# Sums of x for the last three tiles on VectorE in steps 54 to 61, and seven more high halves of weight products on ScalarE

## The reference

```python
# chunked local attention: q, k, v are (4, 8, 768, 64); chunks of 32 queries see 16 keys to the left, 8 to the right, and 8 memory keys
a = softmax(scale * q_c @ k_full.T); out[:, :, c] = a @ v_full
x = out.transpose(0, 2, 1, 3).reshape(3072, 512)
h = x @ w_in0; g = where(h > 0, h, exp(min(h, 0)) - 1); x = g @ w_out0      # layer 1: 512 -> 2048 -> 512
h = x @ w_in1; r = maximum(h, 0); g = s * r * r + b;    x = g @ w_out1      # layer 2, same sizes
```

## Time and profile before

| | us |
|---|---|
| median of three runs | 1180.54 |
| the profiled execution's own time | 1176.55 |
| its span, first to last instruction | 1174.8 |
| attention ahead of step 0 | 97 |
| tile 0 and tile 1 (attention woven in) | 97 to about 526 |
| tile 2, tile 3 | 526 to 688, 688 to 849 |
| tile 4, tile 5 | 849 to 1007, 1007 to 1163 |
| PE, DVE, ACT, POOL busy | 1107.5, 846.0, 769.7, 424.8 |

### The profile page before, as it was taken

How to read it: one execution, slowest core, us unless ns; L and a number is a source line. 1 busy time by engine, 2 the same in 40 slices (tenths; PEclk the granted TensorE clock), 3 DMA queues, 4 the chain that set the end, 5 groups by cost and what they waited for, 6 DMA issues and landing times.

```text
span 1174.8 us, 18155 instructions
## 1 busy us (share of the span) xinstructions
PE 1107.5 (94%) x5787; PEld 881.7 (75%) x5787; DVE 846.0 (72%) x1234; ACT 769.7 (66%) x1799; POOL 424.8 (36%) x458
## 2 busy tenths in 40 slices
PE   8999888988899999999999899998999999999998
PEld 4667566766687777778788687886887887878876
DVE  5786686369957956996948978839948459667385
ACT  4896676577667657757758567666666366675464
POOL 5788778651232332235265233655201001000000
PEclk9999989999999999999999899998999999999999
DMA  9998999999698789869899579996687666776664
GB/s 211 275 267 256 357 290 327 347 297 326 184 286 240 227 242 271 266 191 348 297 356 353 173 255 375 299 349 226 197 249 241 193 194 186 212 222 187 197 183 158
DMA packets 204055, 302.81 MB, mean 258 GB/s; under 512 B 112824, under 2 KB 121016, under 8 KB 203960
## 3 DMA queue, kind: packets, MB, share of 16 engines
q1 hardware_dynamic: 203960, 301.65, 83.8%
HBM read 226.10 MB, written 75.50 MB: 257 GB/s over the span
## 4 chain that ended last, share of the span: by engine, by line
PE 66%; DVE 6%; issue 4%; ACT 3%; DMA 3%; SPq 0%; POOL 0%; ACTq 0%; DVEq 0%; POOLq 0%
PE ps L1010 31%; PE ps L995 31%; DMA w_ring<-w_scratch 2%; ACT ps L1090 1%; DVE g_lo L1450 1%; PE ps L959 1%; DVE X L1367 1%; PE ps L907 1%; PE ps L932 1%; DVE att L1336 1%; DVE xc_lo L1360 1%; DMA elu<-x_scratch 1%; DMA w_raw<-in_moe_w_out 1%; DVE y L1367 1%; PE ps L901 0%
## 5 line engine op out<-in xcount | busy, mean ns | idle before, releaser
L1010 PE MATMUL ps<-g_hi,w_ring 128*128 128x512 f32 x1344 | 426.3, 399 | 22.3 <-issue 16.8
L995 PE MATMUL ps<-xc_hi,w_ring 128*128 128x512 f32 x1344 | 434.0, 396 | 8.4 <-ACT ps L1138 3.3
L1010 PEld LDWEIGHTS ps<-g_hi,w_ring 128*128 128x128 f32 x1344 | 253.5, 192 | 81.6 <-issue 22.4
L995 PEld LDWEIGHTS ps<-xc_hi,w_ring 128*128 128x128 f32 x1344 | 253.1, 188 | 65.4 <-DMA w_ring<-w_scratch 5.3
L1010 PE MATMUL ps<-g_lo,w_ring 128*128 128x512 f32 x672 | 265.1, 395 | 0.0
L995 PE MATMUL ps<-xc_lo,w_ring 128*128 128x512 f32 x672 | 262.4, 391 | 0.0
L782 POOL TENSOR_TENSOR w_new<-w_raw,w_new 128x256 fp32r<-128x256 f32 x182 | 162.4, 896 | 196.3 <-ACT w_new L1227 193.0
L1450 DVE TENSOR_TENSOR g_lo<-X,g_hi 128x512 fp32r<-128x512 f32 x240 | 186.4, 781 | 52.5 <-ACT g_hi L1213 52.0
L1213 ACT ACTIVATE g_hi<-X 128x512 fp32r<-128x512 f32 x240 | 148.8, 627 | 72.5 <-PE ps L1010 66.2
L1367 DVE TENSOR_TENSOR X<-s,ps 128x512 f32<-128x512 f32 x144 | 96.1, 681 | 93.1 <-ACT s L1150 68.5
L1010 PEld LDWEIGHTS ps<-g_lo,w_ring 128*128 128x128 f32 x672 | 128.4, 191 | 27.7
(11 more groups left out here) (116 smaller groups left out, 1388.4 us busy)
## 6 DMA issues: line engine op xcount, KB each, us to landing
w_ring<-w_scratch SPq DMA_DIRECT2D x336, 512.0 KB, 4.4
w_scratch<-w_new SPq DMA_DIRECT2D x182, 256.0 KB, 5.0
w_scratch<-att SPq DMA_DIRECT2D x42, 256.0 KB, 4.9
w_raw<-in_moe_w_in SPq DMA_DIRECT2D x16, 512.0 KB, 5.5
w_raw<-in_moe_w_out SPq DMA_DIRECT2D x16, 512.0 KB, 6.3
x_scratch<-y SPq DMA_DIRECT2D x12, 512.0 KB, 6.4
att<-x_scratch SPq DMA_DIRECT2D x12, 512.0 KB, 6.6
out<-elu SPq DMA_DIRECT2D x24, 256.0 KB, 4.4
```

What stands on the lines that cost most here:

```text
L995: last = nc.tensor.matmul(bank_of(st.pi, st.i), w[:, a, cols], x[:, st.pi, kk, :], start=(st.pi in (P1, P5, P4) and kk == 0 and n == 0), s ...
L1010: last = nc.tensor.matmul(bank_of(st.pi, d), w[:, a, cols], x[:, k % RING, :], start=(st.pi in (P1, P5) + (P4,) * (1 - st.gr) and st.i == ...
```

## The change

HEAD_PREP goes from 42 to 35, so ACT also makes the high halves of products 35 to 41, at steps 7, 7, 8, 9, 10, 11 and 12, and the seven rooms come into use seven products earlier. The slots of the later products are respaced: product 42 goes from step 12 to 13, 49 from 18 to 19, products 56 to 75 stay or move by one, 83 stays at 50, and from there they come up to two steps earlier, the last (111) at 78 instead of 80. The saves due before load d follow: for d = 4 to 9 they were 34, 36, 38, 40, 42, 42 and are 34, 35, 35, 37, 39, 41.

The 24 sums of x for tiles 3 to 5 go from POOL to DVE: in steps 54 to 61 of tiles 2, 3 and 4, one in a step, in the order P5, P7, P6, P4, kk = 0 and 1 in turn. P5 and P4 of kk = 1 get room of their own (`t_more`, 4 KB in each partition), so no sum overwrites a quarter that is still to be split. They stand on DVE behind what the step has otherwise, and in front of the woven attention. POOL then runs straight from set SETS + 4 to the last set.

```diff
-HEAD_PREP = 42
+HEAD_PREP = 35
...
-        return 12 + (pp - HEAD_PREP) * 19 // 20 + (3 if pp >= PREP_AT[PAIR + 1, P1] else 0)
+        return 7 + (pp - HEAD_PREP) * 9 // 10 + (3 if pp >= PREP_AT[PAIR + 1, P1] else 0)
...
+LATE_SUMS = 54
...
+        t_more = sb("t_more", [128, 2, HALF])
...
+        late_sums = sem("late_sums")
...
+        def late_sum(t, kk, pi):
+            return 8 * (t - TPL) + 2 * (SUM_T[pi] - 1) + kk + 1
...
-            if kk == 1 and pi == P6:
-                return t_late[:, 3, :]
+            if kk == 1 and pi in (P5, P6, P4):
+                return {P5: t_more[:, 0, :], P6: t_late[:, 3, :], P4: t_more[:, 1, :]}[pi]
...
-            for m in range(SETS + 4, SETS + 10):
+            for m in range(SETS + 4, 2 * SETS):
                 prepare((m,))
-            for kk in range(2):
-                sums_of_x(3, kk)
-            for m in range(SETS + 10, 2 * SETS):
-                prepare((m,))
-            for t in range(4, TILES):
-                for kk in range(2):
-                    sums_of_x(t, kk)
...
-                if pi not in (P1, P3, P2):
+                if t >= TPL and pi not in (P1, P3, P2):
+                    act.wait_ge(late_sums, late_sum(t, kk, pi))
+                elif pi not in (P1, P3, P2):
...
+            def late_x_sum(t, kk, pi):
+                x11, x12, x21, x22 = (x_from(t, kk, b) for b in (P1, P7, P2, P3))
+                t1, t2, t4 = (x_from(t, kk, b) for b in (P5, P6, P4))
+                if pi == P5:
+                    dve.wait_ge(x_in[kk], 32 * t)
+                    to, a, b = t1, x12, x11
+                elif pi == P7:
+                    dve.wait_ge(late_sums, late_sum(t, kk, P5))
+                    to, a, b = x12, x22, x12
+                elif pi == P6:
+                    dve.wait_ge(late_sums, late_sum(t, kk, P5))
+                    to, a, b = t2, x22, t1
+                else:
+                    dve.wait_ge(late_sums, late_sum(t, kk, P6))
+                    to, a, b = t4, x21, t2
+                nc.vector.tensor_tensor(to, a, b, ALU.subtract).then_inc(late_sums, 1)
...
+                t, s = divmod(g, PER_TILE)
+                if TPL <= t + 1 < TILES and 0 <= s - LATE_SUMS < 8:
+                    late_x_sum(t + 1, (s - LATE_SUMS) % 2, (P5, P7, P6, P4)[(s - LATE_SUMS) // 2])
```

More of the change, by code:

```diff
@@ L809, in sums_of_x @@
                 t1, t2, t4 = (x_from(t, kk, pi) for pi in (P5, P6, P4))
-                late = t >= TPL
-                if kk or not late:
-                    pool.wait_ge(x_lo_done, x_count(t) + x_index(t, kk, P1) + 1)
+                pool.wait_ge(x_lo_done, x_count(t) + x_index(t, kk, P1) + 1)
                 nc.gpsimd.tensor_tensor(t1, x12, x11, ALU.subtract).then_inc(x_sums, 1)
@@ L815, in sums_of_x @@
                 nc.gpsimd.tensor_tensor(x12, x22, x12, ALU.subtract).then_inc(x_sums, 1)
-                if not late:
-                    pool.wait_ge(x_lo_done, x_count(t) + x_index(t, kk, P3) + 1)
-                    pool.wait_ge(x_sums, n + 2)
+                pool.wait_ge(x_lo_done, x_count(t) + x_index(t, kk, P3) + 1)
+                pool.wait_ge(x_sums, n + 2)
                 nc.gpsimd.tensor_tensor(t2, x22, t1, ALU.subtract).then_inc(x_sums, 1)
-                if kk or not late:
-                    pool.wait_ge(x_lo_done, x_count(t) + x_index(t, kk, P2) + 1)
+                pool.wait_ge(x_lo_done, x_count(t) + x_index(t, kk, P2) + 1)
                 pool.wait_ge(x_sums, n + 3)
```

## The result

The changed kernel takes 1164.63 us (median of four runs, 1164.03 to 1168.12), the kernel before 1178.83 beside it: a ratio of 0.9893 (95% interval 0.9853 to 0.9934), which is 12.6 us (7.8 to 17.3); the two medians lie 14.2 us apart. Two later series of the same two kernels gave 1163.05 (0.9870, 0.9852 to 0.9888) and 1165.07 (0.9877, 0.9853 to 0.9902). The forecast was 1163, in a range of 1154 to 1172.

The account below looks back on a forecast made before the run. The prediction took PE, busy 1107.5 of 1174.8 us, as the bound. Moving the sums of x (11.9 us) and seven high halves (3.5) gave 15.4 us off 1178.5, so 1163, in a range of 1154 to 1172.

Parts of the forecast that it names:

- a term that is nothing: Tile 0: moving seven high halves from POOL to ACT gains 3.5 us, with the respacing of cuts costed at nothing.

Follow-up runs that it names:

- the engine without the place: The changed kernel with VectorE's eight sums of x a tile in steps 84 to 91 instead of 54 to 61: 1174.12 us, ratio 0.9970.
- the place without the engine: The changed kernel with the sums of x on GpSimd again, among the weight products of steps 54 to 61 in tiles 2 and 3: 1184.23 us, ratio 1.0047.

## What to carry to other kernels

Ask of every instruction that is moved, even by one step, what it waits for itself and what stands behind it on its engine: a producer that comes early enough for its consumer can still be too early for its own queue. Where GpSimd reads SBUF beside a VectorE that the critical path needs, move the reads to where VectorE is idle, not only to another engine: the engine without the place gave 2 to 4 of the 14 us, and the place without the engine gave nothing (0.5% slower than no change, and level with it without the 6.6 us of tile 4, where POOL didn't keep the place). And when two edits are measured as one, run each alone, since a total that fits can hold a term that is nothing.

## What the runs showed of the hardware

- Beside GpSimd's subtractions of 128x512 a VectorE operation of 128x512 takes 1.2 to 1.75 us in place of 0.68 if both inputs are in SBUF, and 0.67 to 0.68 if one is in PSUM; beside GpSimd's memsets (0.58 us each) it takes 0.68.
- Whether the clock falls is not told by the length of one wait. PE waited 2.52 us ahead of its row at 238.97 before (`<-DVE X L1419`) and kept 1.00 behind it; after, the same wait was 2.54 us and the clock fell to 0.57 in the 4 us behind it, as it did behind the 2.11 us at 226.51. Nor does one kernel always do the same: behind the wait of 1.86 us in steps 0 to 27 of tile 1 the clock fell in seven profiles of fourteen. Why one and not the other these runs don't settle. The row and its window before, and the window after:

```profile
238.97 0.50 PE L995 MATMUL ps<-xc_hi,w_ring 128*128 128x512 f32 x1 [2.52 <-DVE X L1419]
```
```profile
239.00:243.00 4.00, 4.00 (x23) 3.35 (x23) 3.13 (x6) 3.67 (x9) 0.74 (x1) 1.00 0.99 310
```
```profile
244.00:248.00 4.00, 3.99 (x15) 3.27 (x16) 2.19 (x4) 3.16 (x7) 0.00 (x0) 0.57 1.03 368
```
